# A dense layer's gated rows kept in PSUM, with their roundings at a multiple of 128 bytes

## The reference

```python
# attention over 768 positions, 2 x 8 heads of 64: 4 sink keys and a window of 128
a = softmax(where(keep, scale * q @ k.T, -1e9)); x = a @ v          # -> 1536 x 512
# dense layer: 1536 tokens, 512 -> 2048 -> 512
h = x @ w_in
g = h - np.tanh(h)
x = g @ w_out
# mixture of experts: 8 experts, 512 -> 1024 -> 512, the best two of each token
noisy = x @ w_gate + log1p(exp(x @ w_noise)) * noise
out[token] = sum over its two experts e of weight_e * (relu(x @ w1[e]) @ w2[e])
```

## Time and profile before

| | us |
|---|---|
| median of 3 runs | 736.12 (734.84 to 737.18) |
| the profiled execution | 736.07 |
| its span, first to last instruction | 734.0 |
| PE busy | 720.0 (98%) |
| DVE busy | 394.9 (54%) |
| ACT busy | 228.6 (31%) |
| POOL busy | 451.3 (61%) |

### The profile page before, as it was taken

One profiled execution on the slowest core, in us unless ns is written; L12 is line 12 of the kernel. 1 busy time (PEld: TensorE's weight loads), 2 busy tenths in 40 slices (PEclk: granted clock), 3 DMA queues, 4 the chain that ended last, 5 costly groups with the idle time before them and its releaser, 6 DMA issues.

```text
span 734.0 us, 12987 instructions
## 1 busy us (share of the span) xinstructions
PE 720.0 (98%) x3792; PEld 609.3 (83%) x3793; DVE 394.9 (54%) x908; ACT 228.6 (31%) x530; POOL 451.3 (61%) x252
## 2 busy tenths in 40 slices
PE   8999999999999999999979989999999999999998
PEld 6777889989989989989867878888888888888886
DVE  4777554233523442344857647565657565656554
ACT  6999632223222422332223112111212121121112
POOL 6988999000300030003984998949996899987774
PEclk8999999999999999999999999999999999999999
DMA  8742386000100020004345478759785978857776
GB/s 286 268 146 96 114 280 246 0 1 1 73 14 1 0 86 0 0 0 152 120 173 214 126 233 283 256 193 305 245 277 176 321 245 296 271 178 236 236 244 229
DMA packets 69838, 121.46 MB, mean 165 GB/s; under 512 B 8240, under 2 KB 35504, under 8 KB 69296
## 3 DMA queue, kind: packets, MB, share of 16 engines
q1 hardware_dynamic: 28000, 63.92, 25.9%
q10 hardware_dynamic: 37968, 44.58, 17.8%
q0 software_dynamic: 3840, 12.59, 5.3%
HBM read 81.74 MB, written 39.32 MB: 165 GB/s over the span
## 4 chain that ended last, share of the span: by engine, by line
PE 90%; issue 3%; DVE 2%; DMA 2%; POOL 1%; ACT 1%; ACTq 0%; POOLq 0%; DVEq 0%
PE bank L1688 22%; PE bank L1656 22%; PE bank L1513 17%; PE bank L1563 17%; PE bank L1466 4%; PE bank L1457 4%; PE bank L1439 3%; PE bank L1579 1%; DMA hid_lanes<-hid_by_lane 1%; DMA hid_by_lane<-hid 1%; PE bank L1573 1%; DVE gated_lo L1100 1%; DVE arena L1096 0%; ACT gated_hi L861 0%; ACT arena L799 0%
## 5 line engine op out<-in xcount | busy, mean ns | idle before, releaser
L719 POOL DMA_INDIRECT sorted_x<-y_rows,arena x24 | 24.8, 1032 | 211.2 <-DVEq L1177 205.1
L673 POOL TENSOR_TENSOR ring<-ring_raw,ring 128x2048 fp32r<-128x2048 f32 x32 | 148.3, 4633 | 2.5
L1688 PE MATMUL bank<-ring,hidT_hi 128*128 (+1 forms) x448 | 138.4, 390 | 2.4 <-DVE hidT_lo L1261 2.4
L1656 PE MATMUL bank<-ring,xsT_hi 128*128 (+1 forms) x496 | 133.1, 390 | 0.4 <-DVE xsT_lo L1224 0.4
L671 POOL TENSOR_TENSOR ring<-ring_raw,ones 128x2048 fp32r<-128x2048 f32 x32 | 116.3, 3636 | 24.8 <-DMA ring_raw<-in_moe_w 24.7
L1563 PE MATMUL bank<-w_out_sb,gated_hi 128*128 128x512 f32 x384 | 122.4, 400 | 3.5 <-DVE gated_lo L1100 3.5
L1656 PEld LDWEIGHTS bank<-ring,xsT_hi 128*128 128x128 f32 x496 | 92.7, 188 | 19.9 <-issue 0.8
L1688 PEld LDWEIGHTS bank<-ring,hidT_hi 128*128 128x128 f32 x448 | 83.8, 188 | 20.2 <-issue 3.0
L1096 DVE TENSOR_TENSOR arena<-bank,arena 128x384 f32<-128x384 f32 x64 | 35.6, 556 | 105.4 <-ACT arena L856 104.2
L1688 PE MATMUL bank<-ring,hidT_lo 128*128 (+1 forms) x224 | 87.2, 389 | 0.0
L1513 PE MATMUL bank<-xT_hi,w_in_hi 128*128 (+1 forms) x256 | 87.0, 340 | 0.0
(11 more groups left out here) (205 smaller groups left out, 1069.0 us busy)
## 6 DMA issues: line engine op xcount, KB each, us to landing
ring_raw<-in_moe_w SPq DMA_DIRECT2D x48, 512.0 KB, 5.4
hid_by_lane<-hid ACTq DMA_DIRECT2D x28, 512.0 KB
hid_lanes<-hid_by_lane ACTq DMA_DIRECT2D x28, 512.0 KB
ring_raw<-in_moe_w SPq DMA_DIRECT2D x8, 1024.0 KB, 7.1
sorted_y<-ys ACTq DMA_DIRECT2D x31, 256.0 KB
xs<-sorted_x ACTq DMA_DIRECT2D x100, 64.0 KB
sorted_y<-zeros SPq DMA_DIRECT2D x1, 4864.0 KB, 26.2
arena<-in_k SPq DMA_DIRECT2D x8, 520.0 KB, 4.7
```

Source lines behind the costliest of these rows:

```text
L673: ins = pool.tensor_tensor(lo, raw, hi.bitcast(F32), ALU.subtract)
L1656: last = pe.matmul(bank[banks + half][:, :], x[:, c * P:(c + 1) * P], ring[:, bass.ds(at * 2 * WE + (w + c * FE + half * BANK), BANK)], st ...
L1688: last = pe.matmul(bank[into][:, :], x[:, c * P:(c + 1) * P], ring[:, bass.ds(at * 2 * WE + (w + CH * FE + c * DM), DM)], start=c == 0 and ...
```

## The change

The buffer `gated` is gone. DVE writes `bank - tanh_h` back into the bank that it read (L1096); ACT rounds from the bank (L861), and DVE's second subtraction takes the bank and `gated_hi` (L1100). The bank is therefore in use until that second subtraction, and PE waits before `hidden(fc)` for `gated_split` of chunk fc - 2 instead of `gated_ready`, the semaphore for which `project(fc - 2)`, next in its queue, waits anyway.

The start of the arena's part for this layer is rounded up to a multiple of 32 columns. `gated_hi` and `gated_lo` begin at column 52512, a multiple of 128 bytes, and `tanh_h` and `x2T` behind and ahead of them at such multiples too. No instruction is added, removed or put in another place on any engine.

```diff
         behind_routing = used[0]
 
+        used[0] = -(-used[0] // 32) * 32
+        assert ARENA % 32 == 0
         tanh_h = [part([BLK]) for u in range(2)]
-        gated = [part([BLK]) for u in range(2)]
         G = 3
         gated_at = ARENA + used[0]
...
                 act.wait_ge(gated_ready, blk * FC + fc + 1)
-                act.copy(gated_hi[fc % G][:, :], gated[fc % 2][:, :]).then_inc(gated_rounded, 1)
+                act.copy(gated_hi[fc % G][:, :], bank[fc % 2][:, 0:BLK]).then_inc(gated_rounded, 1)
...
                 dve.wait_ge(tanh_ready, blk * FC + fc + 1)
-                dve.tensor_tensor(gated[fc % 2][:, :], bank[fc % 2][:, 0:BLK], tanh_h[fc % 2][:, :],
+                dve.tensor_tensor(bank[fc % 2][:, 0:BLK], bank[fc % 2][:, 0:BLK], tanh_h[fc % 2][:, :],
                                   ALU.subtract).then_inc(gated_ready, 1)
 
                 dve.wait_ge(gated_rounded, blk * FC + fc + 1)
-                dve.tensor_tensor(gated_lo[fc % G][:, :], gated[fc % 2][:, :], gated_hi[fc % G][:, :].bitcast(F32),
+                dve.tensor_tensor(gated_lo[fc % G][:, :], bank[fc % 2][:, 0:BLK], gated_hi[fc % G][:, :].bitcast(F32),
                                   ALU.subtract).then_inc(gated_split, 1)
...
                 if fc >= 2:
 
-                    pe.wait_ge(gated_ready, blk * FC + fc - 1)
+                    pe.wait_ge(gated_split, blk * FC + fc - 1)
```

## The result

Over 12 runs the changed kernel takes 730.69 us (726.67 to 733.45), the kernel before, in 12 runs, 735.38 (731.12 to 740.29). The ratio is 0.9938 (95% interval 0.9914 to 0.9961): 4.7 us faster, where 10.3 were forecast. The profiled execution of after took 733.36 us, with a span of 731.4.

A forecast was written before the change was run, and what follows sets the result against it. PE, busy for 98% of the span, was taken to bound the kernel. From the profiled 736.07 us, 3.5 (lock), 1.5 (clock) and 5.3 (alignment) were taken off, giving 725.8 us; range 724.0 to 732.0.

The forecast's parts named there:

- The alignment: Dense layer: with gated_hi and gated_lo at multiples of 128 bytes, project reaches down's pace, 3.8 us; with hidden, 5.3.
- rival 1: Project's extra 20 ns per matmul belong to something other than the place; only lock and clock gained, 731.1 us; chance 0.22.
- hidden's part: The slow first half of hidden, seen only behind a project, goes too: 0.027 us in some 55 chunks, 1.5 us.
- The lock: End of block 3: L1100, reading the bank, is no longer held by POOL's splits; both PE waits go, 3.5 us.
- rival 2: L1100 is held all the same because gated_hi still comes from SBUF; alignment alone counts, 730.8 us; chance 0.06.
- The clock: project(15), end of block 3: without PE's waits the low clock at 374 us goes, 3.58 to 2.10, 1.5 us.
- In place: Dense layer: L1096 writing to PSUM and L861 reading it are covered by PE's own work, worth nothing.
- the later wait: PE's wait before hidden(fc) for gated_split costs 0, since project(fc - 2) would wait for the same semaphore anyway.
- Rival 4: PE's PSUM writes suffer from the new traffic, 9.0 us slower, giving 740.1 us; chance 0.05.
- The shift is therefore passed on whole: From 378 us on, everything is released by PE or what it releases, so the dense layer's gain reaches the end.

The follow-up runs named there:

- bank alone: Changed kernel without the rounding up, gated_hi again 96 bytes past a multiple of 128: 731.56 us against 731.62 for the kernel before, ratio 0.9996.
- place alone: Kernel before with only the arena's start rounded up, gated staying in SBUF: 729.63 us against 731.62 for the kernel before, ratio 0.9978.
- The three comparisons: Unaltered changed kernel measured three times against the kernel before, 12 runs each time: ratios 0.9938, 0.9965 and 0.9962.
- second comparison: Changed kernel measured again, nothing altered, against the kernel before: 729.0 us (12 runs) against 731.62 (35 runs), ratio 0.9965.

## Why the forecast went wrong, step by step

**"The alignment", project's part, 3.8 us: the mechanism held, the size did not.** Project's 20 ns do hang on the place of the stationary operand: in a run of 27 each matmul takes 233 ns at 96 bytes past a multiple of 128 (before, bank alone), and 227 at a multiple from the tenth on (after, place alone). The chains at block 3's end in the second profile of before and in the first of after:

```profile
366.37 6.30 PE bank L1563 x27
```

```profile
364.65 6.17 PE bank L1564 x27
```

The rule of the Trainium skill that spoke against it, page "Advanced Engine Details and Errata", section "Memory Cachelines" (lines of 16 bytes), would have given no difference; the two experiments show 1.5 us in the dense layer, so here the measurement decides. But I carried down's pace to a group of nine matmuls, when down had shown it in groups of 24 between groups with the same number of columns. In project it is reached only behind the slow start: 2.10 - 2.08 = 0.02 us per chunk where a hidden comes ahead (13 in each of four blocks, 1.0 us) and 0.14 us in the 27 in a row at each block's end (6.30 to 6.16, 0.6 us). That is 1.6 us instead of 3.8. The forecast had its warning in view: rival 1 noted that down too has slow starts behind an idle PE.

**"The alignment", hidden's part, 1.5 us ("as if PE first had to catch up on what the project cost"): wrong.** Its halves are 1.07 and 1.04 us with either place, and the slow one vanished when the columns were made equal. That term was 0.

**"The lock", 3.5: right in mechanism, wrong as a fixed cost of the kernel.** L1101 is never held, and rival 2 falls with it. The Trainium skill, page "SBUF — State Buffer", section "SBUF: two separate sides", says that a VectorE operation with two SBUF inputs and a GpSimd operation that reads SBUF shut each other out for a whole instruction. The traces agree: 3.80 us with two SBUF inputs beside POOL, 558 ns with one in PSUM. But the two waits stood in one of three executions of before. The step that failed is to have made the sum against a single profiled execution and taken its waits for fixed ones. The median beside it hid this, since it was 0.05 us from that execution; whether the other runs had the same waits or other losses in their place, no trace shows.

**"The clock", 1.5: wrong.** "If PE does not stand still, I see nothing that would take the clock away" failed: it fell within 6 us of there in two profiles of after and in two of before that had no such wait. Nor do blocks 1 to 3 stand for the end of block 3, as the prediction had it: there each routing step has a hidden ahead of it, while behind block 3 all three follow each other, 4.5 to 5.1 us of transposes and 16-column matmuls alone. The low clock is a cost behind that stretch in some executions and not in others; what decides, no run shows, and none shows that the change touches it.

**"In place" and "the later wait", 0: right.** L1097 takes 566 ns instead of 556, L862 takes 481 instead of 515, and PE never waited for `gated_split` ahead of a hidden. Rival 4 falls: with the new PSUM traffic the dense layer takes 286.8 us, without it (place alone) 286.9.

**"The shift is therefore passed on whole": not to be read from one execution.** From the end of the dense layer to the last down the three profiles of after took 357.2, 355.1 and 351.8 us, the three of before 352.8, 352.9 and 354.4. Of the 4.4 us given back, 1.6 are the low clock, which in before fell into project(15), 1.9 the handing over to the experts (up to down(3)), and 0.9 the last two downs. In the handing over the chain runs through DMAs that scatter. In the first profile of after:

```profile
418.01 8.64 DMA hid_by_lane<-hid
426.67 7.15 DMA hid_lanes<-hid_by_lane
```

and in the third:

```profile
414.68 7.00 DMA hid_by_lane<-hid
421.70 6.47 DMA hid_lanes<-hid_by_lane
```

PE waited 1.95 us behind the first pair (at 437.34), 0.28 behind the second (at 431.75). In before the pair took 6.66 and 8.40 us and PE waited 1.52, so this place explains only part of the 1.9. The spread of 5.4 us between executions of one program is larger than all that the change brings.

**What the change is worth.** The dense layer shows 1.6 us (288.4 to 286.8), nearly all by the place. The three comparisons give 2.5 to 4.7, with intervals some 3 us wide; 1.6 us lies inside the second and the third and outside the first. The difference of one to three us would fit executions of before that had waits like those of its first profile; how often it has them was not measured, and in the second comparison the bank, which ends such waits, gave 0.1 us by itself and the place 2.0. So that part stays open. 730.69 lies within the forecast's range, near rivals 1 and 2, but neither is what happened: the place counts, for less than was forecast, and the waits are there only in some executions. That the number fell into the range is luck.

## What to carry to other kernels

A wait that one profile shows at the meeting of two engines with different periods may be chance, as here: profile the kernel two or three times before its waits enter a sum, and look whether the awaited operation's length depends on when it starts. Down's pace, read from groups of 24, held for project's groups of nine only when the group ahead had the same number of columns; where two shapes alternate, count the changes. And read what a change saves between two fixed marks around its stage, since what lies behind them scattered here by 5 us.

## What the hardware showed that I had not expected

- The first matmuls behind a change of the number of columns are slow in both directions: nine of 512 columns behind 384 take 2.08 us instead of 2.04, twelve of 384 behind 512 some 30 ns more than at their later pace, and 18 of 512 take the same 40 ns more as nine.
- The stationary operand's place modulo 128 bytes costs 6 ns per matmul of 512 columns (233 against 227) at 96 bytes past a multiple, from the tenth matmul behind the change of columns on; in the first nine the two places differ by 0.02 us in all. Other places were not tried.
- A DVE subtraction with two SBUF inputs that starts while POOL runs an SBUF operation ends 0.40 to 0.42 us behind POOL's, so it takes 0.6 to 3.8 us by its phase, and in one execution six in a row were held for 2.8 to 3.8 us behind a chunk that came 1.0 us late.
- The clock falls to 1.2 GHz for 3.41 or 6.83 us behind the last routing in some executions of one program and not in others (two of three of the changed kernel), at 1.6 us for each 3.41.
